# Row-split output matmuls and transposes, and d_ff blocks taken one by one, in a dynamic-convolution and SwiGLU kernel

## The chip, the cores and the metric

The kernel runs on one core of one Trainium2 chip. The time is the device time of one execution in microseconds (us); before the change it was 1409.2 us (median of three runs, 1408.73 to 1409.4).

## What is computed

The reference, cut to what matters:

```python
# x: (4, 4096, 192), weight_gen: (4, 4096, 8 heads, 7 taps)
w = softmax(weight_gen, axis=-1)                 # over the 7 taps
x_pad = six rows of zeros ahead of each sequence
out[b, s, h, g] = sum_k w[b, s, h, k] * x_pad[b, s + k, h*24 + g]
# then, on the 16384 rows of out (d_model 192, d_ff 1536):
xn  = x / sqrt(mean(x*x) + 1e-6) * rms_g
g   = xn @ w_gate ; val = xn @ w_val
return (g * sigmoid(g) * val) @ w_out
```

## The kernel before

**Tiles and blocks.** The 16384 tokens are cut into 32 tiles T of 512 tokens (J = 4 groups of 128). d_ff is cut into FB = 12 blocks f of 128 columns. For each tile and block TensorE does two things:

- `hidden(T, t, f)`, called H(f) below, makes gate and val of the block, transposed: 128 d_ff columns by 512 tokens. The contraction over 192 channels is held in SLOTS = 3 slots of 64 rows, and each operand is split into a high and a low part (float32r), with the three products high-high, low-high, high-low. So H(f) is 9 pairs of matmuls. In each pair the gate matmul uses rows 0 to 63 of the array and the val matmul rows 64 to 127; they write different PSUM banks.
- `project(T, f)`, called P(f), adds the block to the output: for each group j of 128 tokens a matmul of the high part of h with 384 columns (high and low part of w_out side by side) and one of its low part with 192 columns, both over all 128 rows, into the group's own bank of `out_ps`. That is 8 matmuls.

**The chain between them.** ScalarE makes `silu` from gate (L414); VectorE multiplies it with val to h (L538); ScalarE copies the high part `h_hi` (L419); VectorE subtracts to `h_lo` (L556). P(f) waits for `h_lo`. gate and val have two banks each, so H(f+2) waits until h of block f is made.

**Turning x.** Once a tile, `turn_x` transposes the normalised tokens of the next tile on TensorE into a free bank (4 and 2 transposes of 128x128 against the identity). ScalarE copies the high part out (`x_high`, L382 and L385), VectorE the low part (`x_low`, L474 and L478), and three DMAs copy halves between the partitions. The H two blocks later needs that bank again.

**Other work.** VectorE also makes the convolution of the tile after the next in 17 steps (`mix`, two lines L192 and L194 with 0.95 us a step for most), dealt out over the blocks by `steps_other`. ScalarE squares and scales tokens. GpSimd makes 1/rms. In the first tiles VectorE takes the maxima of the remaining taps (L515) and GpSimd subtracts them (L314).

**Order.** Each engine's order is written out by hand, with semaphores; nothing reorders it. On TensorE blocks come in twos: H(f), H(f+1), P(f-2), P(f-1). `turn_x` stands between the two P of f = 4 (`turn_after` is 5). The first H of a tile is followed by H(1), then P(10) and P(11) of the tile before.

Of the kernel before, what the change touches and what calls it, by code (L numbers as in the profile page):

```python
# [5 lines left out]
ALU = mybir.AluOpType  # L6
# [10 lines left out]
def dynconv_swiglu(nc, x, weight_gen, w_gate, w_val, w_out, rms_g, out):  # L17
# [17 lines left out]
    DB = D - DA  # L35
    SLOTS = D // DB
    CHUNKS = ((0, 1, 2), (1, 0, 2))
    FIRST = 3
# [12 lines left out]
    with ExitStack() as ctx:  # L51
# [44 lines left out]
        h = sb("h", [P, 2, N])  # L96
        h_hi = sb("h_hi", [P, 3, N], F32R)
        h_lo = sb("h_lo", [P, 3, N], F32R)
# [42 lines left out]
        h_lo_done = sem("h_lo_done")  # L141
        out_mm_done = sem("out_mm_done")
        out_part_done = sem("out_part_done")
# [9 lines left out]
        def turn_after(T):  # L153


            return 9 if isinstance(T, int) and T == 0 else 5

# [5 lines left out]
        pieces = [slice(a * J * H, b * J * H) for a, b in zip(cuts, cuts[1:])]  # L163

        def rest_to(t, part, odd):

            return xT[0:DB, t, 2, part, :].rearrange("p (j o c) -> p j o c", o=2, c=P)[:, :, odd, :]

        def rest_of(banks, odd):

            return val_ps[odd * DB:odd * DB + DB, banks, 0:N // 2].rearrange("p (j c) -> p j c", c=P)

# [163 lines left out]
        def _(act):  # L336
# [22 lines left out]
            def square(T, t, js):  # L359
                if isinstance(T, int) and T < 2:  # L360
                    act.wait_ge(first_mix, FIRST_DONE)
                    act.wait_ge(pool_mix, CONV * (T + 1))
                else:
                    act.wait_ge(mix_steps, MIX * (T - 1))
                if not (isinstance(T, int) and T == 0):

                    act.wait_ge(mean_done, T)
                    act.wait_ge(xT_done, 2 * T)
# [28 lines left out]
            def out_low(T):  # L397


                act.wait_ge(out_mm_done, FB * (T + 1))  # L400
                nc.scalar.activation(out_part, out_ps[:, :, D:2 * D], ACT.Copy).then_inc(out_part_done, 1)  # L401

            def tile(T, t, first=False, last=False, exps=()):
                xf = turn_after(T)
                squares_at, scales_at = (xf - 4, xf - 3) if first else (0, 2), (xf - 2, xf - 1) if first else (3, 4)
                for f in range(FB):
                    b = pair(t, step_of(f, xf))
                    if f == 2 and not first:
# [5 lines left out]
                    nc.scalar.activation(silu[:, f % 2, :], gate_ps[:, b, :], ACT.Silu).then_inc(silu_done, 1)  # L414
                    act.wait_ge(h_done, FB * T + f + 1)
                    if not (first and f < 3):
# [11 lines left out]
                    if f == xf:  # L428
                        x_high(T + 1, 1 - t, pair(t, xf + 1))
# [16 lines left out]
        def _(dve):  # L446
# [25 lines left out]
            def x_low(T, t, banks):  # L472
                dve.wait_ge(x_hi_done, 3 * T + 1)
                nc.vector.tensor_tensor(xT[:, t, 0, 1, :], gate_ps[:, banks, :], xT[:, t, 0, 0, :].bitcast(F32),  # L474
                                        ALU.subtract).then_inc(x_lo_done, 1)
                for odd in range(2):
                    dve.wait_ge(x_hi_done, 3 * T + 2 + odd)
                    nc.vector.tensor_tensor(rest_to(t, 1, odd), rest_of(banks, odd), rest_to(t, 0, odd).bitcast(F32),  # L478
# [50 lines left out]
            def tile(T, t, i, first=False, mixes=True, last=False):  # L529
                xf = turn_after(T)  # L530
                steps = steps_first if first else steps_other
                for f in range(FB):
                    b = pair(t, step_of(f, xf))
                    if f == 2 and not first:
                        out_add(T - 1, 1 - t, None if isinstance(T, int) and T < 3 else 16 * (i - (1 - t)))
# [7 lines left out]
                    if mixes:  # L543
                        for n in range(sum(steps[:f]), sum(steps[:f + 1])):
# [10 lines left out]
                    dve.wait_ge(h_hi_done, FB * T + f + 1)  # L555
                    nc.vector.tensor_tensor(h_lo[:, f % 3, :], h[:, f % 2, :], h_hi[:, f % 3, :].bitcast(F32),  # L556
                                            ALU.subtract).then_inc(h_lo_done, 1)
                    if f == xf and not last:
                        x_low(T + 1, 1 - t, pair(t, xf + 1))

            tile(0, 0, 0, first=True)
# [11 lines left out]
        def _(pe):  # L573
            def turn_x(T, t, banks):


                pe.wait_ge(xn_done, 2 * J * (T + 1))
                for j in range(J):
                    mm = nc.tensor.transpose(gate_ps[:, banks, j * P:(j + 1) * P], xn_a[:, j, :], ident[:])  # L579
                mm.then_inc(xT_done, 1)  # L580
                for j in range(0, J, 2):
                    mm = nc.tensor.transpose(val_ps[:, banks, j // 2 * P:(j // 2 + 1) * P], xn_b[:, j:j + 2, :].rearrange("p j d -> p (j d)"), ident[:])  # L582
                mm.then_inc(xT_done, 1)
# [44 lines left out]
            def project(T, f):  # L628

                pe.wait_ge(h_lo_done, FB * T + f + 1)  # L630
                for j in range(J):
                    cols = slice(j * P, (j + 1) * P)
                    nc.tensor.matmul(out_ps[:, j, 0:2 * D], h_hi[:, f % 3, cols], wo[:, f, :, :].rearrange("p a d -> p (a d)"),  # L633
                                     start=(f == 0), stop=False, skip_group_check=True)
                    mm = nc.tensor.matmul(out_ps[:, j, 0:D], h_lo[:, f % 3, cols], wo[:, f, 0, :],  # L635
                                          start=False, stop=(f == FB - 1), skip_group_check=True)
                mm.then_inc(out_mm_done, 1)

            def tile(T, t, first=False, last=False):
                xf = turn_after(T)  # L640
                for f in range(0, FB, 2):
                    hidden_waits(T, f, first)
                    hidden(T, t, f)
                    if not (last and f + 1 == xf + 2):
                        hidden_waits(T, f + 1, first)
                    hidden(T, t, f + 1)
                    if f == 0:
                        if not first:
                            project(T - 1, FB - 2)
                            project(T - 1, FB - 1)  # L650
                        continue
                    if f == 2:
# [18 lines left out]
            for _ in range(WARM_TURNS):  # L671
                nc.tensor.transpose(gate_ps[:, 0, 0:P], ident[:], ident[:])
            turn_x(0, 0, 1)
# [30 lines left out]
```

## Time and profile before

| what | value |
|---|---|
| median of 3 runs | 1409.2 us |
| the profiled execution | 1406.67 us, its span 1404.9 us |
| TensorE busy | 1357.4 us, 97% of the span |
| VectorE busy | 996.9 us, 71% |
| ScalarE busy | 659.3 us, 47% |
| mean granted TensorE clock | 0.99 |

The span goes from the first to the last instruction. A matmul's row has a start and a duration; matmuls are pipelined, so the next one starts well before the one before has ended. What a matmul costs a busy TensorE is therefore the distance from its start to the next start. Two matmuls on different halves of the rows start together and count as one step.

### The profile page before, as it was taken

How to read it: one execution, taken by the hardware profiler on the slowest of the kernel's cores; microseconds unless marked ns; L12 is line 12 of the kernel's file. 1: busy time of each engine (PE TensorE's matmuls, PEld its weight loads, DVE VectorE, ACT ScalarE, POOL GpSimd, SP SyncE). 2: the span in 40 equal slices, each digit the busy share in tenths (PEclk: the TensorE clock that was granted, in tenths of full speed). 3: DMA queues.
4: the chain of work that ended last, by engine and by line, in shares of the span. 5: the costliest groups of instructions: out<-in, count | busy, mean ns of one | idle time of the engine just before them, and what ended most of it. 6: DMA issues, size and time to landing. Idle time of an engine off the chain costs nothing.

```text
span 1404.9 us, 27539 instructions
## 1 busy us (share of the span) xinstructions
PE 1357.4 (97%) x10260; PEld 1121.2 (80%) x10260; DVE 996.9 (71%) x1438; ACT 659.3 (47%) x1427; POOL 106.6 (8%) x104
## 2 busy tenths in 40 slices
PE   4898899999999999999999999999999999999998
PEld 3676678888888888888888888888888888888887
DVE  6786777777777777777777777777777777777543
ACT  4354464444444444444444444444444444544443
POOL 7710200000000000000000000000000000000000
PEclk9899999999999999999999999999999999999999
DMA  9121112111211211211211221211121221120010
GB/s 300 24 63 44 42 40 63 51 40 56 62 43 58 62 50 34 62 56 45 62 50 34 62 62 39 62 50 37 59 62 39 62 62 44 40 62 23 22 35 12
DMA packets 20009, 76.19 MB, mean 54 GB/s; under 512 B 3215, under 2 KB 5007, under 8 KB 19854
## 3 DMA queue, kind: packets, MB, share of 16 engines
q1 hardware_dynamic: 19982, 75.83, 18.1%
q8 instruction: 16, 0.26, 0.1%
q14 instruction: 11, 0.09, 0.0%
HBM read 38.07 MB, written 12.58 MB: 36 GB/s over the span
## 4 chain that ended last, share of the span: by engine, by line
PE 92%; DVE 4%; issue 2%; ACT 1%; DMA 1%; POOL 0%; SPq 0%; POOLq 0%; DVEq 0%; ACTq 0%
PE gate_ps L609 56%; PE out_ps L633 23%; PE out_ps L635 9%; PE val_ps L609 2%; PE gate_ps L579 1%; DVE h L538 1%; DVE prod L192 1%; DVE y L194 1%; PE val_ps L582 0%; DVE h_lo L556 0%; DVE tap_max L515 0%; ACT silu L414 0%; ACT xn L377 0%; DMA xT<-xT 0%; DMA taps<-in_weight_gen 0%
## 5 line engine op out<-in xcount | busy, mean ns | idle before, releaser
L609 PE MATMUL gate_ps<-xT,w_hi 64*128 64x512 f32 x2304 | 774.9, 402 | 11.6 <-DMA xT<-xT 5.4
L609 PE MATMUL val_ps<-xT,w_hi 64*128 64x512 f32 x2304 | 775.3, 403 | 0.0
L609 PEld LDWEIGHTS gate_ps<-xT,w_hi 64*128 64x128 f32 x2304 | 427.5, 186 | 137.0 <-issue 33.0
L538 DVE TENSOR_TENSOR h<-val_ps,silu 128x512 f32<-128x512 f32 x384 | 265.1, 690 | 343.3 <-ACT silu L414 343.2
L633 PE MATMUL out_ps<-wo,h_hi 128*128 128x384 f32 x1536 | 474.3, 372 | 0.0
L609 PE MATMUL val_ps<-xT,w_lo 64*128 64x512 f32 x1152 | 453.8, 394 | 0.0
L609 PE MATMUL gate_ps<-xT,w_lo 64*128 64x512 f32 x1152 | 453.4, 394 | 0.0
L609 PEld LDWEIGHTS val_ps<-xT,w_hi 64*128 64x128 f32 x2304 | 427.5, 186 | 0.8
L419 ACT ACTIVATE h_hi<-h 128x512 fp32r<-128x512 f32 x384 | 242.9, 632 | 369.3 <-DVE h L538 369.3
L414 ACT ACTIVATE silu<-gate_ps 128x512 f32<-128x512 f32 x384 | 227.5, 593 | 349.1 <-PE gate_ps L609 339.1
L635 PE MATMUL out_ps<-wo,h_lo 128*128 128x192 f32 x1536 | 385.1, 251 | 0.0
L633 PEld LDWEIGHTS out_ps<-wo,h_hi 128*128 128x128 f32 x1536 | 289.6, 189 | 69.6 <-issue 69.6
L556 DVE TENSOR_TENSOR h_lo<-h,h_hi 128x512 fp32r<-128x512 f32 x384 | 268.8, 700 | 37.2 <-ACT h_hi L419 37.2
L635 PEld LDWEIGHTS out_ps<-wo,h_lo 128*128 128x128 f32 x1536 | 294.3, 192 | 0.0
L609 PEld LDWEIGHTS gate_ps<-xT,w_lo 64*128 64x128 f32 x1152 | 214.4, 186 | 39.0
L609 PEld LDWEIGHTS val_ps<-xT,w_lo 64*128 64x128 f32 x1152 | 214.4, 186 | 0.4
L194 DVE TENSOR_TENSOR y<-y,prod 128x768 f32<-128x768 f32 (+1 forms) x186 | 186.8, 1004 | 2.3
L192 DVE TENSOR_TENSOR prod<-x_buf,tap_w 128x768 f32<-128x768 f32 x180 | 171.1, 951 | 1.1
L283 POOL TENSOR_TENSOR mean_sq<-sq_mean,eps_rms 128x4 f32<-128x4 f32 x32 | 17.6, 550 | 1205.8 <-ACT xn L370 1205.8
L377 ACT ACTIVATE xn<-y,inv_rms 128x128 f32<-128x128 f32 (+1 forms) x256 | 74.0, 360 | 4.4 <-POOL inv_rms L285 4.4
L370 ACT ACTIVATE xn<-y 128x192 f32<-128x192 f32 x128 | 44.4, 348 | 1.7 <-DVE y L194 1.7
L522 DVE TENSOR_TENSOR last<-out_ps,last 128x768 f32<-128x768 f32 x32 | 30.6, 958 | 6.6 <-ACT last L401 3.4
(47 smaller groups left out, 431.9 us busy)
## 6 DMA issues: line engine op xcount, KB each, us to landing
x_buf<-in_x SPq DMA_DIRECT2D x30, 960.0 KB, 4.6
xT<-xT SPq DMA_DIRECT2D x96, 256.0 KB, 3.8
result<-last SPq DMA_DIRECT2D x32, 384.0 KB, 2.3
taps<-in_weight_gen SPq DMA_DIRECT2D x1, 3248.0 KB, 19.5
raw<-in_moe_w_gate SPq DMA_DIRECT2D x3, 384.0 KB, 6.5
raw<-in_moe_w_val SPq DMA_DIRECT2D x3, 384.0 KB, 7.6
last<-in_moe_w_out SPq DMA_DIRECT2D x1, 1152.0 KB, 12.6
x_first<-in_x SPq DMA_DIRECT2D x2, 384.0 KB, 4.9
```

The source lines that it names most:

```text
L192: return engine.tensor_tensor(heads(product if n else acc), heads(flat(src[:, k + j0:k + j1, :])), w[:, q0:q1, k].unsqueeze(2).to_broadcas ...
L194: return engine.tensor_tensor(acc, acc, product, ALU.add)
L370: nc.scalar.activation(xn[:, j * D:(j + 1) * D], y[:, t, j, :], ACT.Square, scale=D ** -0.5, accum_out=sq_mean[:, j:j + 1]).then_inc(squar ...
L377: nc.scalar.activation(part[:, j, :], y[:, t, j, d], ACT.Copy, scale=inv_rms[:, j:j + 1]).then_inc(xn_done, 1)
L414: nc.scalar.activation(silu[:, f % 2, :], gate_ps[:, b, :], ACT.Silu).then_inc(silu_done, 1)
L419: nc.scalar.activation(h_hi[:, f % 3, :], h[:, f % 2, :], ACT.Copy).then_inc(h_hi_done, 1)
L522: nc.vector.tensor_tensor(out_sb[:, t, :, :], out_ps[:, :, 0:D], out_part, ALU.add).then_inc(out_added, 1)
L538: nc.vector.tensor_tensor(h[:, f % 2, :], val_ps[:, b, :], silu[:, f % 2, :], ALU.mult).then_inc(h_done, 1)
L556: nc.vector.tensor_tensor(h_lo[:, f % 3, :], h[:, f % 2, :], h_hi[:, f % 3, :].bitcast(F32), ALU.subtract).then_inc(h_lo_done, 1)
L609: mm = nc.tensor.matmul(ps[:, banks, :], w[rows, s, cols], xT[rows, t, s, part, :], start=(s == 0 and n == 0), stop=ends)
L633: nc.tensor.matmul(out_ps[:, j, 0:2 * D], h_hi[:, f % 3, cols], wo[:, f, :, :].rearrange("p a d -> p (a d)"), start=(f == 0), stop=False, ...
L635: mm = nc.tensor.matmul(out_ps[:, j, 0:D], h_lo[:, f % 3, cols], wo[:, f, 0, :], start=False, stop=(f == FB - 1), skip_group_check=True)
```

## The change

The output matmuls are split in two by rows: rows 0 to 63 of the block go to one group j of tokens and, beside them, rows 64 to 127 to group j + 2, in four turns k = 0 to 3; in turn k + 2 the halves change places. Both halves add into the same bank of `out_ps`, two turns apart, and a new semaphore `bank_left` keeps them apart: turn n waits until all matmuls of turn n - 2 have ended. The transposes are split in the same way (12 instead of 6, with 64 columns each), and write the banks of gate and val, which are now one tensor `up_ps`. Blocks are taken one by one: H(f), P(f-2). `turn_x` moves one block later (`turn_after` is 6), after H(6) and P(4) and ahead of P(5); H(7) then follows without a P between. `h_hi` and `h_lo` have four buffers instead of three. ScalarE's `x_high` stands ahead of the block's `h_hi`, and VectorE's `x_low` ahead of its `h_lo`, and `x_low` now begins after all three copies of `x_high`. Squares, scales, `out_low` and `out_add` come one block earlier.

```diff
+    HB = 4
-        gate_ps = psum("gate_ps", [P, 2, N])
-        val_ps = psum("val_ps", [P, 2, N])
+        up_ps = psum("up_ps", [P, 2, 2, N])
+        gate_ps, val_ps = up_ps[:, :, 0, :], up_ps[:, :, 1, :]
...
-            return 9 if isinstance(T, int) and T == 0 else 5
+            return 9 if isinstance(T, int) and T == 0 else 6
...
             def x_high(T, t, banks):
-                act.wait_ge(xT_done, 2 * T + 1)
-                nc.scalar.activation(xT[:, t, 0, 0, :], gate_ps[:, banks, :], ACT.Copy).then_inc(x_hi_done, 1)
-                act.wait_ge(xT_done, 2 * T + 2)
+                act.wait_ge(xT_done, T + 1)
+                nc.scalar.activation(main_to(t, 0), main_of(banks), ACT.Copy).then_inc(x_hi_done, 1)
...
-                squares_at, scales_at = (xf - 4, xf - 3) if first else (0, 2), (xf - 2, xf - 1) if first else (3, 4)
+                squares_at, scales_at = (xf - 4, xf - 3) if first else (0, 1), (xf - 2, xf - 1) if first else (2, 3)
...
-                        act.wait_ge(out_mm_done, FB * T + f - 2)
-                    nc.scalar.activation(h_hi[:, f % 3, :], h[:, f % 2, :], ACT.Copy).then_inc(h_hi_done, 1)
+                        act.wait_ge(bank_left, 2 * J * (FB * T + f - HB + 1))
+                    nc.scalar.activation(h_hi[:, f % HB, :], h[:, f % 2, :], ACT.Copy).then_inc(h_hi_done, 1)
...
             def x_low(T, t, banks):
-                dve.wait_ge(x_hi_done, 3 * T + 1)
+                dve.wait_ge(x_hi_done, 3 * T + 3)
...
             def turn_x(T, t, banks):
-                pe.wait_ge(xn_done, 2 * J * (T + 1))
                 for j in range(J):
-                    mm = nc.tensor.transpose(gate_ps[:, banks, j * P:(j + 1) * P], xn_a[:, j, :], ident[:])
-                mm.then_inc(xT_done, 1)
...
+                    for m in range(2):
+                        rows = slice(m * DB, (m + 1) * DB)
+                        mm = nc.tensor.transpose(up_ps[:, banks, m, j * DB:(j + 1) * DB], xn_a[rows, j, :], ident[rows, rows])
...
             def project(T, f):
                 pe.wait_ge(h_lo_done, FB * T + f + 1)
-                for j in range(J):
-                    cols = slice(j * P, (j + 1) * P)
-                    nc.tensor.matmul(out_ps[:, j, 0:2 * D], h_hi[:, f % 3, cols], wo[:, f, :, :].rearrange("p a d -> p (a d)"),
-                                     start=(f == 0), stop=False, skip_group_check=True)
-                    mm = nc.tensor.matmul(out_ps[:, j, 0:D], h_lo[:, f % 3, cols], wo[:, f, 0, :],
-                                          start=False, stop=(f == FB - 1), skip_group_check=True)
-                mm.then_inc(out_mm_done, 1)
+                for k in range(J):
+                    turn = J * FB * T + J * f + k
+                    if not (isinstance(turn, int) and turn < 2):
+                        pe.wait_ge(bank_left, 2 * (turn - 1))
+                    for m in range(2):
+                        j = (k + 2 * m) % J
+                        rows, cols = slice(m * DB, (m + 1) * DB), slice(j * P, (j + 1) * P)
+                        nc.tensor.matmul(out_ps[:, j, 0:2 * D], h_hi[rows, f % HB, cols],
+                                         wo[rows, f, :, :].rearrange("p a d -> p (a d)"),
+                                         start=(f == 0 and k < 2), stop=False, skip_group_check=True)
+                    for m in range(2):
+                        j = (k + 2 * m) % J
+                        rows, cols = slice(m * DB, (m + 1) * DB), slice(j * P, (j + 1) * P)
+                        nc.tensor.matmul(out_ps[:, j, 0:D], h_lo[rows, f % HB, cols], wo[rows, f, 0, :], start=False,
+                                         stop=(f == FB - 1 and k >= 2), skip_group_check=True).then_inc(bank_left, 1)
...
-                for f in range(0, FB, 2):
-                    hidden_waits(T, f, first)
-                    hidden(T, t, f)
...
-                    project(T, f - 2)
-                    if f + 1 == xf and not last:
...
-                        turn_x(T + 1, 1 - t, pair(t, xf + 1))
-                    project(T, f - 1)
+                for f in range(FB):
...
+                    if 2 <= f <= xf or f > xf + 1:
+                        project(T, f - 2)
+                    if f == xf:
+                        if not last:
+                            turn_x(T + 1, 1 - t, pair(t, xf + 1))
+                        project(T, xf - 1)
```

TensorE's queue before, where H of a tile's block 5 ends and P(2) begins (L609 is H, L633 and L635 are P, L577 to L582 belong to `turn_x`; the names in brackets are the semaphores waited for):

```order
L609 MATMUL gate_ps<-xT,w_hi 128x512
L609 MATMUL val_ps<-xT,w_hi 128x512
L633 MATMUL out_ps<-wo,h_hi 128x384 [waits h_lo_done]
L635 MATMUL out_ps<-wo,h_lo 128x192
L633 MATMUL out_ps<-wo,h_hi 128x384
```

The queue of the changed kernel, where an H ends and a P begins, up to its turn k = 2 (L619 is H, L649 and L655 are P; ISA is a register instruction):

```order
L619 MATMUL up_ps<-xT,w_hi 128x512 x2
L645 ISA [waits h_lo_done]
L649 MATMUL out_ps<-wo,h_hi 128x384 [waits bank_left]
L649 MATMUL out_ps<-wo,h_hi 128x384
L655 MATMUL out_ps<-wo,h_lo 128x192 x2
L645 ISA
L649 MATMUL out_ps<-wo,h_hi 128x384 [waits bank_left]
L649 MATMUL out_ps<-wo,h_hi 128x384
L655 MATMUL out_ps<-wo,h_lo 128x192 x2
L645 ISA
L649 MATMUL out_ps<-wo,h_hi 128x384 [waits bank_left]
```

Four matmuls now stand where two stood, and each turn begins with a wait of TensorE for its own earlier matmuls.

ScalarE's queue before, around the copies of the turned x of a tile (L382, L385):

```order
L414 ACTIVATE silu<-gate_ps 128x512 [waits h_done,gate_done]
L419 ACTIVATE h_hi<-h 128x512 [waits out_mm_done,h_done]
L382 ACTIVATE xT<-gate_ps 128x512 [waits xT_done]
L385 ACTIVATE xT<-val_ps 64x2x128 [waits xT_done]
L385 ACTIVATE xT<-val_ps 64x2x128
```

The same place of the changed kernel (L391, L393):

```order
L422 ACTIVATE silu<-up_ps 128x512 [waits h_done,gate_done]
L391 ACTIVATE xT<-up_ps 128x512 [waits xT_done]
L393 ACTIVATE xT<-up_ps 64x2x128 x2
L429 ACTIVATE h_hi<-h 128x512 [waits bank_left,h_done]
L422 ACTIVATE silu<-up_ps 128x512 [waits h_done,gate_done]
```

The copies of x have moved ahead of the copy of h, and wait for all transposes at once.

## Rows read from the trace of the kernel before

**Rows 1.** The profile page, busy time and share of the engines.
```profile
PE 1357.4 (97%) x10260; PEld 1121.2 (80%) x10260; DVE 996.9 (71%) x1438; ACT 659.3 (47%) x1427; POOL 106.6 (8%) x104
```

**Rows 2.** The chain that ended last, by engine (page).
```profile
PE 92%; DVE 4%; issue 2%; ACT 1%; DMA 1%; POOL 0%; SPq 0%; POOLq 0%; DVEq 0%; ACTq 0%
```

**Rows 3.** Busy time in one tile's stretch: us, then busy (count) per engine, clock, DMA.
```profile
686.33:728.08 41.75, 41.75 (x321) 34.53 (x319) 30.40 (x46) 19.77 (x44) 1.53 (x2) 1.00 0.17 52
```

**Rows 4.** Timeline of TensorE, end of a P, start of an H: start, us.
```profile
702.28 0.25 PE L635 MATMUL out_ps<-wo,h_lo 128*128 128x192 f32 x1
702.46 0.49 PE L609 MATMUL gate_ps<-xT,w_hi 64*128 64x512 f32 x1
...
702.80 0.39 PE L609 MATMUL gate_ps<-xT,w_lo 64*128 64x512 f32 x1
...
703.03 0.40 PE L609 MATMUL gate_ps<-xT,w_hi 64*128 64x512 f32 x1
```

**Rows 5.** Timeline of TensorE, end of an H, start of a P.
```profile
706.53 0.39 PE L609 MATMUL gate_ps<-xT,w_hi 64*128 64x512 f32 x1
...
706.86 0.45 PE L633 MATMUL out_ps<-wo,h_hi 128*128 128x384 f32 x1
707.14 0.25 PE L635 MATMUL out_ps<-wo,h_lo 128*128 128x192 f32 x1
707.23 0.36 PE L633 MATMUL out_ps<-wo,h_hi 128*128 128x384 f32 x1
707.42 0.25 PE L635 MATMUL out_ps<-wo,h_lo 128*128 128x192 f32 x1
```

**Rows 6.** Timeline of TensorE around the transposes of x.
```profile
708.00 0.25 PE L635 MATMUL out_ps<-wo,h_lo 128*128 128x192 f32 x1
708.08 0.60 PE L579 MATMUL gate_ps<-ident,xn 128*128 128x128 f32 x4
708.52 0.38 PE L582 MATMUL val_ps<-ident,xn 128*128 128x128 f32 x2
708.66 0.42 PE L633 MATMUL out_ps<-wo,h_hi 128*128 128x384 f32 x1
```

**Rows 7.** Timeline of weight loads at the start of an H.
```profile
702.46 0.18 PEld L609 LDWEIGHTS gate_ps<-xT,w_hi 64*128 64x128 f32 x1 [0.16 <-issue]
702.47 0.18 PEld L609 LDWEIGHTS val_ps<-xT,w_hi 64*128 64x128 f32 x1
702.57 0.19 PEld L609 LDWEIGHTS gate_ps<-xT,w_lo 64*128 64x128 f32 x1
702.57 0.19 PEld L609 LDWEIGHTS val_ps<-xT,w_lo 64*128 64x128 f32 x1
```

**Rows 8.** Timeline where TensorE is woken by another engine (tile 0).
```profile
78.11 0.86 DVE L478 TENSOR_TENSOR xT<-val_ps,xT 64x256 fp32r<-64x256 f32 x2
...
79.03 0.18 PEld L609 LDWEIGHTS gate_ps<-xT,w_hi 64*128 64x128 f32 x1 [1.26 <-DVE xT L478]
```

**Rows 9.** The same in tile 1, with a wait for two semaphores.
```profile
130.46 0.69 DVE L538 TENSOR_TENSOR h<-val_ps,silu 128x512 f32<-128x512 f32 x1 [3.91 <-ACT silu L414]
...
131.27 0.18 PEld L609 LDWEIGHTS gate_ps<-xT,w_hi 64*128 64x128 f32 x1 [2.12 <-ACT silu L414]
```

**Rows 10.** Timelines of ScalarE, VectorE and TensorE after a turn of x.
```profile
709.69 0.58 ACT L382 ACTIVATE xT<-gate_ps 128x512 fp32r<-128x512 f32 x1
710.16 0.77 ACT L385 ACTIVATE xT<-val_ps 64x256 fp32r<-64x256 f32 x2
...
710.50 0.68 DVE L474 TENSOR_TENSOR xT<-gate_ps,xT 128x512 fp32r<-128x512 f32 x1
711.10 0.86 DVE L478 TENSOR_TENSOR xT<-val_ps,xT 64x256 fp32r<-64x256 f32 x2
...
712.16 0.40 PE L609 MATMUL gate_ps<-xT,w_hi 64*128 64x512 f32 x1
```

**Rows 11.** The chain that ended last in tile 1: start, us, what.
```profile
97.07 2.86 DVE tap_max L515
...
100.86 5.43 issue
```

**Rows 12.** The stretch at half clock in tile 1, columns as in Rows 3.
```profile
107.40:114.30 6.90, 4.85 (x20) 4.40 (x22) 5.15 (x9) 3.93 (x10) 0.00 (x0) 0.51 0.00 0
```

More of the change, by code:

```diff
@@ L96, in dynconv_swiglu @@
         h = sb("h", [P, 2, N])
-        h_hi = sb("h_hi", [P, 3, N], F32R)
-        h_lo = sb("h_lo", [P, 3, N], F32R)
+        h_hi = sb("h_hi", [P, HB, N], F32R)
+        h_lo = sb("h_lo", [P, HB, N], F32R)
         out_part, out_sb = last[:, 0, :, :], last[:, 1:3, :, :]
-        gate_ps = psum("gate_ps", [P, 2, N])
-        val_ps = psum("val_ps", [P, 2, N])
+        up_ps = psum("up_ps", [P, 2, 2, N])
+        gate_ps, val_ps = up_ps[:, :, 0, :], up_ps[:, :, 1, :]
         out_ps = psum("out_ps", [P, J, N])
@@ L367, in square @@
                     act.wait_ge(mean_done, T)
-                    act.wait_ge(xT_done, 2 * T)
+                    act.wait_ge(xT_done, T)
                 for j in js:
@@ L404, in tile @@
                 xf = turn_after(T)
-                squares_at, scales_at = (xf - 4, xf - 3) if first else (0, 2), (xf - 2, xf - 1) if first else (3, 4)
+                squares_at, scales_at = (xf - 4, xf - 3) if first else (0, 1), (xf - 2, xf - 1) if first else (2, 3)
                 for f in range(FB):
                     b = pair(t, step_of(f, xf))
-                    if f == 2 and not first:
+                    if f == 1 and not first:
                         out_low(T - 1)
@@ L414, in tile @@
                     nc.scalar.activation(silu[:, f % 2, :], gate_ps[:, b, :], ACT.Silu).then_inc(silu_done, 1)
+                    if f == xf and not last:
+                        x_high(T + 1, 1 - t, pair(t, xf + 1))
                     act.wait_ge(h_done, FB * T + f + 1)
-                    if not (first and f < 3):
-                        act.wait_ge(out_mm_done, FB * T + f - 2)
-                    nc.scalar.activation(h_hi[:, f % 3, :], h[:, f % 2, :], ACT.Copy).then_inc(h_hi_done, 1)
+                    if not (first and f < HB):
+                        act.wait_ge(bank_left, 2 * J * (FB * T + f - HB + 1))
+                    nc.scalar.activation(h_hi[:, f % HB, :], h[:, f % 2, :], ACT.Copy).then_inc(h_hi_done, 1)
                     if last:
@@ L427, in tile @@
                         scale(T + 1, 1 - t, range(2 * n, 2 * n + 2))
-                    if f == xf:
-                        x_high(T + 1, 1 - t, pair(t, xf + 1))
                     for at, n in exps:
@@ L533, in tile @@
                     b = pair(t, step_of(f, xf))
-                    if f == 2 and not first:
+                    if f == 1 and not first:
                         out_add(T - 1, 1 - t, None if isinstance(T, int) and T < 3 else 16 * (i - (1 - t)))
@@ L554, in tile @@
                             mix(T + 2, t, n)
-                    dve.wait_ge(h_hi_done, FB * T + f + 1)
-                    nc.vector.tensor_tensor(h_lo[:, f % 3, :], h[:, f % 2, :], h_hi[:, f % 3, :].bitcast(F32),
-                                            ALU.subtract).then_inc(h_lo_done, 1)
                     if f == xf and not last:
                         x_low(T + 1, 1 - t, pair(t, xf + 1))
+                    dve.wait_ge(h_hi_done, FB * T + f + 1)
+                    nc.vector.tensor_tensor(h_lo[:, f % HB, :], h[:, f % 2, :], h_hi[:, f % HB, :].bitcast(F32),
+                                            ALU.subtract).then_inc(h_lo_done, 1)
             tile(0, 0, 0, first=True)
@@ L574, in turn_x @@
             def turn_x(T, t, banks):
-                pe.wait_ge(xn_done, 2 * J * (T + 1))
                 for j in range(J):
-                    mm = nc.tensor.transpose(gate_ps[:, banks, j * P:(j + 1) * P], xn_a[:, j, :], ident[:])
-                mm.then_inc(xT_done, 1)
-                for j in range(0, J, 2):
-                    mm = nc.tensor.transpose(val_ps[:, banks, j // 2 * P:(j // 2 + 1) * P], xn_b[:, j:j + 2, :].rearrange("p j d -> p (j d)"), ident[:])
+                    for m in range(2):
+                        rows = slice(m * DB, (m + 1) * DB)
+                        mm = nc.tensor.transpose(up_ps[:, banks, m, j * DB:(j + 1) * DB], xn_a[rows, j, :], ident[rows, rows])
+                for q in range(J // 2):
+                    for m in range(2):
+                        rows = slice(m * DB, (m + 1) * DB)
+                        mm = nc.tensor.transpose(up_ps[:, banks, m, N // 2 + q * DB:N // 2 + (q + 1) * DB],
+                                                 xn_b[rows, 2 * q:2 * q + 2, :].rearrange("p j d -> p (j d)"), ident[rows, rows])
                 mm.then_inc(xT_done, 1)
@@ L639, in tile @@
             def tile(T, t, first=False, last=False):
                 xf = turn_after(T)
-                for f in range(0, FB, 2):
-                    hidden_waits(T, f, first)
+                for f in range(FB):
+                    if not (last and f == xf + 2):
+                        hidden_waits(T, f, first)
                     hidden(T, t, f)
[L644 to L651, printed above, removed]
+                    if f == 0 and not first:
+                        project(T - 1, FB - 2)
+                        project(T - 1, FB - 1)
@@ L657, in tile @@
                             pe.wait_ge(w_lo_done, SLOTS + 1)
-                    project(T, f - 2)
-                    if f + 1 == xf and not last:
+                    if f == xf and not last:
                         pe.wait_ge(silu_done, FB * T + xf)
                         pe.wait_ge(h_done, FB * T + xf)
-                        turn_x(T + 1, 1 - t, pair(t, xf + 1))
-                    project(T, f - 1)
+                        pe.wait_ge(xn_done, 2 * J * (T + 2))
+                    if 2 <= f <= xf or f > xf + 1:
[4 more added lines that the diff above has]
+                        project(T, xf - 1)
             pe.wait_ge(consts_done, 1)
@@ L671, in _ @@
             for _ in range(WARM_TURNS):
-                nc.tensor.transpose(gate_ps[:, 0, 0:P], ident[:], ident[:])
+                nc.tensor.transpose(up_ps[:, 0, 0, 0:P], ident[:], ident[:])
+            pe.wait_ge(xn_done, 2 * J)
             turn_x(0, 0, 1)
```

16 lines of the change are left out of this document (10 added, 6 removed).

## The prediction

> **What bounds the kernel now.** I read the page's busy times first: TensorE is busy for 97% of the span, VectorE for 71%, ScalarE for 47% [rows 1]. The chain that ended last says the same: 92% of the span goes through TensorE [rows 2]. One tile in the steady part takes 41.75 us, at full clock, and TensorE has no idle time in it, while VectorE works 30.40 us and ScalarE 19.77 us [rows 3]. So the time is what TensorE's instructions cost from start to start, and the other engines matter only where they make it wait. That happens in the first tiles (below).
>
> Now the steps, from start to start. Inside an H a pair takes 0.233 us: one starts at 702.80, the next at 703.03, and from 702.80 to the last pair at 706.53 there are 16 steps [rows 4, 5]. Inside a P the step after an h_hi matmul is 0.19 and after an h_lo matmul 0.09; from 707.14 to 708.00 three groups of tokens pass, 0.286 each [rows 5, 6]. Transposes and the step into them show nothing extra: 0.08 after the h_lo matmul at 708.00, and about 0.65 us for all six, of which 0.58 lie between 708.08 and 708.66 [rows 6]. So a tile should need 12 x 9 x 0.233 = 25.2, 12 x 4 x 0.286 = 13.7, and 0.65: 39.5 us. It takes 41.75. The missing 2.2 us are at the borders between H and P, of which there are six there and six back in a tile. Going to H: 0.18 instead of 0.09, then 0.34 instead of 0.233 [rows 4]. Going to P: 0.33 instead of 0.233, then 0.28 instead of 0.19 [rows 5]. Together 0.38 us for a round trip, and 2.2 / 6 = 0.37 from the tile. What is special there is that the number of rows changes, 64 to 128 or back. P to transposes and back, 128 rows throughout, shows none of it, and neither does H to H.
>
> **The change, part by part.**
>
> *Borders.* With P and the transposes on 64 rows, no border between different row counts is left. I take the whole 2.2 us off each tile: 32 x 2.2 = 70.4 us. That there are now 12 round trips a tile instead of 6 then costs nothing. The Trainium skill says, in TensorEngine Tiling (Array Packing), Tiling Modes, that changing the tiling mode drains TensorE. The trace agrees in the place of the gaps; the skill gives no time for it.
>
> *The split matmuls.* A P had 8 matmuls and 8 loads, now 16 and 16, in 8 steps of two. Columns per step are as before. What must hold is that the loads and matmuls of two row halves run side by side also when the steps are as short as 0.09. H shows matmuls side by side, but its steps are long. For the loads the best rows are the start of an H: gate and val load at 702.46 and 702.47, and the next two both at 702.57, so two loads per half, four in all, start within 0.11 us [rows 7]. Had they gone through one port one by one, the second pair would start at 0.2 and 0.3 us. I take 0.286 for a turn, as before. The bound on the good side is the same; on the bad side it is a rival below.
>
> *The wait for the bank.* Turn n waits for all of turn n - 2. The second h_lo matmul of a turn starts 0.01 after the first and lasts 0.25 [rows 5]; TensorE's load starts 0.06 after the end of the VectorE instruction that it waits for (78.11 + 0.86 = 78.97, load at 79.03) [rows 8]. So turn k + 2 can load 0.32 after turn k's h_lo step starts. Without the wait its load would stand at the start of turn k + 1's h_lo step, 0.286 later. It is 0.034 late at least. In a P that follows an H, turns 0 and 1 wait for turns long past; turn 2 pays, and turn 3 hardly, since turn 1 is judged against a stream that turn 2 has already set back. So one payment a block. I take 0.06 us, as the rows are rounded, two semaphore counts must arrive and a register instruction stands ahead of each wait: 384 x 0.06 = 23 us. The bounds: nothing (0 us), if the queue holds enough, and 0.12 us with the dearer wake of [rows 9], where 131.15 to 131.27 is 0.12 and not 0.06, plus 0.03 for refilling: 46 us. Queued behind a waiting turn are only TensorE's own matmuls. By the Trainium skill, TensorE: Matmul & The Clock Gate, Part 3 on the per-tile semaphore tail, each further increment adds 26.3 ns; an estimate with it is 0.034 + 0.026 = 0.06 us a block. No row here shows that figure.
>
> *Blocks one by one.* H(f+2) needs h of block f. Between the end of H(f) and the start of H(f+2) now lie P(f-2), H(f+1) and P(f-1), 1.2 + 2.1 + 1.2 = 4.5 us, while silu and h take 0.6 and 0.69 and a short wait for the matmul's end: covered by some 2 us even when VectorE first finishes a 0.95 step and an h_lo. P(f) comes after H(f+2), later still. VectorE's 30.4 us [rows 3] lie inside a tile of 40.3 us. I cost this at nothing. Without its cover it would cost what the VectorE is late, up to a step of 0.95 a block.
>
> *The turned x.* H(8) needs the low part of x. From the first transpose: 0.82 to the end of the last (708.52 + 0.38 - 708.08) [rows 6]; then x_high 1.24 (709.69 to 710.93) and, now only after it, x_low 0.60 + 0.86 = 1.46 [rows 10]; with three hand-overs of 0.05, 3.65 us. Before, ScalarE began 1.61 after the first transpose, held by h_hi, and the low part was done at 711.96, 0.20 ahead of the H at 712.16 [rows 10]. H(8) now starts 0.65 + 4 x 0.286 + 0.06 + 9 x 0.233 = 3.95 us after the first transpose. The slack stays, 0.3 us. I cost it at nothing; if the copies, whose pieces are now 64 columns wide, took 30% longer, 0.8 us, H(8) would be 0.5 late in 31 tiles: 16 us. The halves' DMAs have the rest of the tile. In tile 0 x_low starts about 0.7 later and the first H with it.
>
> *The first tiles.* In tiles 1 and 2 a reduction of 2.86 us and then 5.43 us in which VectorE stands still hold up h, and through h the normalised x [rows 11]; the transposes wait 6 us and the clock is 0.51 for 6.9 us afterwards [rows 12]. These waits are set by VectorE and GpSimd, and P(3) will meet them instead of the transposes. One block less has been issued ahead of it, but P(3) needs less than the transposes did. Between -2 and +8 us, I take 2 us gained in all.
>
> *Sum.* Against the profiled execution: 1406.7 - 70.4 + 23 - 2 = 1357.3 us. The median is 2.5 above that execution, so 1360 us, a tile of 12 x (2.10 + 1.14 + 0.06) + 0.65 = 40.3 us.
>
> **The rivals.**
>
> *The wait is free.* The queue is deep enough and the wake quick: the 23 us are not paid, perhaps more is won in the first tiles: 1337 us. For it: only 0.034 us is missing. Against: the load cannot start before its wait ends.
>
> *The wait is dear,* or every border to H refills TensorE's queue, or H(8) is late: 0.12 to 0.17 a block, 46 to 65 us instead of 23: 1383 to 1402 us. For it: 16 instructions, register steps and waits now share 1.2 us.
>
> *The short steps don't run side by side.* Place: each turn of P. If the two halves' loads take turns, the h_lo step lasts two loads, 2 x 0.11 = 0.22 instead of 0.09, and the h_hi step 0.22 instead of 0.19: 0.16 more a turn, 384 x 4 x 0.16 = 246 us: 1360 + 246, about 1606 us. It decides from (70.4 - 23 + 2) / 1536 = 0.03 us a turn. Against it stand the loads of [rows 7]; for it, that no row shows steps under 0.23 with two halves.
>
> *The borders are not of the row count* but of any change from H to P, for instance queue refills. Then 12 round trips instead of 6 cost 70 us more: 1409 + 70 + 23 = 1502 us. Against it: the borders at the transposes cost nothing.
>
> *VectorE's latency shows.* Stalls of 0.5 to 2 us a tile: 1376 to 1420 us. A tile leaves VectorE 10 us free [rows 3], so I hold it small.
>
> **How the numbers follow.** Forecast 0.54 (its own range 1346 to 1380); wait free 0.15; wait dear 0.13; not side by side 0.07; borders remain 0.04; VectorE's latency 0.07, half of that still faster. Faster by over 0.2% (which is about what a measurement of this kernel can tell) is 0.54 + 0.15 + 0.13 + 0.04 = 0.86; slower 0.12; same 0.02. The range that holds eight in ten takes in the first three cases, from 1334 (all of the wait free, 2 us more in the first tiles) to 1395.
>
> **What the profile after would show.** Right: starts across a border 0.23 and 0.09 apart; a turn of 0.286 from turn 0 to 1 and some 0.06 more into turn 2; a tile of 40.3 us with no TensorE idle time; H(8) right after H(7). Wrong: turns over 0.32 from the first on (halves not side by side); 0.33 at H to P as now (borders not of the row count); VectorE or ScalarE as releasers of H(8), or of H in every tile; a second gap at the P to H border (queue refill).

## The result, and the profile after

The changed kernel takes 1415.1 us (median of five runs, 1413.1 to 1416.0) against 1408.7 us before: a ratio of 1.0045, 95% interval 1.003 to 1.006. It is slower by half a per cent, where 1360 us had been forecast. Its profiled execution has a span of 1411.3 us. All ratios here and below are taken from executions in the faster of two states; one execution of experiment 5 fell in the slower one, with 1401.9 us at a mean granted clock of 0.845, and is not counted.

The page, lines that answer to [rows 1], and the queue that fetches instructions:

```profile
PE 1319.6 (94%) x13524; PEld 1146.7 (81%) x13524; DVE 1002.0 (71%) x1438; ACT 660.3 (47%) x1427; POOL 97.2 (7%) x104
...
q8 instruction: 138, 2.26, 0.7%
```

TensorE has more instructions than before (13524 matmuls instead of 10260), less busy time, and is now idle for 6% of the span instead of 3%. The last line (packets, MB, share) had 16 packets and 0.26 MB before.

First the part that was forecast. TensorE's timeline from the last pair of an H through a P into the next H, which answers to [rows 4, 5] (start, us):

```profile
701.65 0.40 PE L619 MATMUL up_ps<-xT,w_hi 64*128 64x512 f32 x2
701.89 0.34 PE L649 MATMUL out_ps<-wo,h_hi 64*128 64x384 f32 x2
702.06 0.25 PE L655 MATMUL out_ps<-wo,h_lo 64*128 64x192 f32 x2
702.15 0.36 PE L649 MATMUL out_ps<-wo,h_hi 64*128 64x384 f32 x2
702.35 0.25 PE L655 MATMUL out_ps<-wo,h_lo 64*128 64x192 f32 x2
702.43 0.41 PE L649 MATMUL out_ps<-wo,h_hi 64*128 64x384 f32 x2
702.68 0.25 PE L655 MATMUL out_ps<-wo,h_lo 64*128 64x192 f32 x2
702.77 0.36 PE L649 MATMUL out_ps<-wo,h_hi 64*128 64x384 f32 x2
702.97 0.25 PE L655 MATMUL out_ps<-wo,h_lo 64*128 64x192 f32 x2
703.05 0.42 PE L619 MATMUL up_ps<-xT,w_hi 64*128 64x512 f32 x2
703.31 0.39 PE L619 MATMUL up_ps<-xT,w_lo 64*128 64x512 f32 x2
...
706.33 0.42 PE L619 MATMUL up_ps<-xT,w_hi 64*128 64x512 f32 x2
```

H to P takes 0.24 us, where it took 0.33; P to H 0.08 and then 0.26, where it took 0.18 and 0.34. Turns 0 and 1 take 0.26 and 0.28. Turn 2 begins on time at 702.43, but its first step lasts 0.25 instead of 0.20: its load, at 702.40, starts 0.05 after the h_lo matmuls of 702.35, where turn 1's load, at 702.07, starts 0.01 after those of 702.06. A block takes 3.28 us, from the H at 703.05 to the one at 706.33; 3.30 had been forecast. A tile without a pause takes 39.89 us at full clock (the same pair of H starts at 313.71 and, a tile later, at 353.60), with TensorE busy throughout. The first row below covers all but 0.09 us of it and answers to [rows 3]; the one after it answers to [rows 12]:

```profile
314.00:353.80 39.80, 39.80 (x422) 34.56 (x420) 30.64 (x45) 19.77 (x44) 1.21 (x2) 1.00 0.12 31
394.80:398.90 4.10, 3.75 (x20) 3.37 (x22) 0.00 (x0) 0.00 (x0) 0.00 (x0) 0.60 0.49 204
```

Now the part that was not. Every second tile ends like this:

```profile
391.33 0.36 PE L649 MATMUL out_ps<-wo,h_hi 64*128 64x384 f32 x2
391.53 0.25 PE L655 MATMUL out_ps<-wo,h_lo 64*128 64x192 f32 x2
395.15 0.50 PE L619 MATMUL up_ps<-xT,w_hi 64*128 64x512 f32 x2 [3.37 <-issue]
395.46 0.56 PE L619 MATMUL up_ps<-xT,w_lo 64*128 64x512 f32 x2
```

TensorE stands still for 3.37 us, and no other engine or DMA of the program is named as releaser, that is, as what ended the wait ("issue" stands there instead). Behind most of these pauses the clock is at its lower level for 3.4 us or twice that: 0.60 is the mean of the stretch above. The profile's list of waits counts the pauses (us in total, times, longest):

```profile
PE up_ps L619 <- issue: 44.3, 13, 3.7
```

Thirteen pauses, 44.3 us, 3.7 at most. Thirteen is the number of times that TensorE's loop over pairs of tiles jumps back. The instructions at the source line of the loop show the jump itself. PEldq is the sequencer that feeds TensorE, COMPARE_BRANCH the jump (count: shortest, median, longest in ns). In the kernel before:

```profile
L676 PEldq COMPARE_BRANCH  x14: 76/208/242, 227.1 to 1312.7; - x14
```

and in the changed kernel:

```profile
L696 PEldq COMPARE_BRANCH  x14: 83/3422/3777, 222.8 to 1323.4; - x14
```

Thirteen jumps of 3.3 to 3.8 us, the last one (not taken) 0.08. Before the change they took 0.21, and TensorE did not stand still: its queue still held matmuls. Counted in the traces, the loop's body on TensorE had 1333 instructions before (636 loads, 636 matmuls, 61 others) and has 1839 now (840, 840, and 159, of which 96 are the register instructions ahead of the bank waits).

**Theory A:** the body no longer stays in TensorE's instruction store, the memory into which its instructions are fetched, and each jump back waits until its first instructions have been fetched again; with the clock that is what ate the gain. **Theory B:** the pause belongs to the new order or to a wait for another engine at the start of a pair of tiles, and the long branch only covers it.

### The profile page after: what moved, and what is told of

Read it like the earlier page. It is cut to its first block, busy times and chain, and to the rows that moved or that the text cites. A ratio compares the mean times of both kernels' runs of the same rounds, so it can differ in the third digit from the quotient of the medians.

```text
span 1411.3 us, 35391 instructions
## 1 busy us (share of the span) xinstructions
PE 1319.6 (94%) x13524; PEld 1146.7 (81%) x13524; DVE 1002.0 (71%) x1438; ACT 660.3 (47%) x1427; POOL 97.2 (7%) x104
## 4 chain that ended last, share of the span: by engine, by line
PE 88%; issue 4%; DVE 4%; ACT 3%; DMA 1%; POOL 0%; SPq 0%; ACTq 0%; POOLq 0%
PE up_ps L619 57%; PE out_ps L649 21%; PE out_ps L655 9%; DVE h L545 1%; ACT silu L422 1%; DMA xT<-xT 1%; DVE prod L201 1%; PE up_ps L587 1%; DVE y L203 1%; DVE tap_max L522 0%; ACT taps L403 0%; ACT xn L386 0%; DVE h_lo L565 0%; DMA taps<-in_weight_gen 0%; PE up_ps L591 0%
## 5 line engine op out<-in xcount | busy, mean ns | idle before, releaser
L619 PE MATMUL up_ps<-xT,w_hi 64*128 64x512 f32 x4608 | 800.4, 402 | 53.9 <-issue 44.3
L619 PEld LDWEIGHTS up_ps<-xT,w_hi 64*128 64x128 f32 x4608 | 445.4, 188 | 146.3 <-issue 48.5
L649 PE MATMUL out_ps<-wo,h_hi 64*128 64x384 f32 x3072 | 488.2, 370 | 12.7 <-DVE h_lo L565 12.7
L545 DVE TENSOR_TENSOR h<-up_ps,silu 128x512 f32<-128x512 f32 x384 | 265.3, 691 | 300.0 <-ACT silu L422 292.1
L619 PE MATMUL up_ps<-xT,w_lo 64*128 64x512 f32 x2304 | 464.3, 397 | 0.0
L422 ACT ACTIVATE silu<-up_ps 128x512 f32<-128x512 f32 x384 | 227.9, 594 | 377.5 <-PE up_ps L619 375.4
L655 PE MATMUL out_ps<-wo,h_lo 64*128 64x192 f32 x3072 | 391.1, 250 | 0.0
L649 PEld LDWEIGHTS out_ps<-wo,h_hi 64*128 64x128 f32 x3072 | 295.8, 187 | 42.5 <-issue 8.7
L655 PEld LDWEIGHTS out_ps<-wo,h_lo 64*128 64x128 f32 x3072 | 298.6, 189 | 13.8
L619 PEld LDWEIGHTS up_ps<-xT,w_lo 64*128 64x128 f32 x2304 | 223.9, 189 | 36.5
L391 ACT ACTIVATE xT<-up_ps 128x512 fp32r<-128x512 f32 x32 | 19.2, 599 | 30.7 <-PE up_ps L591 30.7
```

What stands on the lines that cost most here:

```text
L545: nc.vector.tensor_tensor(h[:, f % 2, :], val_ps[:, b, :], silu[:, f % 2, :], ALU.mult).then_inc(h_done, 1)
L619: mm = nc.tensor.matmul(ps[:, banks, :], w[rows, s, cols], xT[rows, t, s, part, :], start=(s == 0 and n == 0), stop=ends)
L649: nc.tensor.matmul(out_ps[:, j, 0:2 * D], h_hi[rows, f % HB, cols], wo[rows, f, :, :].rearrange("p a d -> p (a d)"), start=(f == 0 and k < ...
L655: nc.tensor.matmul(out_ps[:, j, 0:D], h_lo[rows, f % HB, cols], wo[rows, f, 0, :], start=False, stop=(f == FB - 1 and k >= 2), skip_group_ ...
```

## The experiments

**1. The loop written out.** Edit on the changed kernel:

```diff
-            with pe.Fori(1, TILES // 2 - 1) as i:
+            for i in range(1, TILES // 2 - 1):
                 tile(2 * i, 0)
```

> The changed kernel with TensorE's loop over pairs of tiles written out in full (the other engines keep their loops). Theory A (code fetch): the 13 taken branches back, 3.3 to 3.8 us each, and the stretch at half clock behind each, some 1.6 us, are the cost of fetching the first instructions of a loop body that no longer fits. Without a branch both go: 13 x 5.1 = 67 us less than the changed kernel, 1348 us, no gap over 1 us between the H of tiles 4 and 28. Theory B (a wait for another engine or a DMA at the start of an odd-even pair of tiles): the gap stays, the time stays at 1415 us.

Measured: 1352.9 us, ratio to the kernel before 0.9599 (0.9583 to 0.9616). The pauses are gone; all tiles from 3 on take 40.13 us. Its fetch queue moves 108 packets, 1.77 MB, nearly as much as in the changed kernel, and nothing waits: straight code is fetched ahead, so the traffic is not the cost. Theory B falls; the size of the body, theory A's reason, is tested in experiments 3, 8 and 9.

**2. The loop kept, with a hint:** one instruction at the loop's top that names the jump back and its target.

```diff
-            with pe.Fori(1, TILES // 2 - 1) as i:
+            with nc.Fori(1, TILES // 2 - 1, engines=[mybir.EngineType.PE], hint_back_edge=True) as i:
```

> The changed kernel, its loop kept, with one hint instruction at the top of TensorE's loop that names the branch back and its target. Theory A: the first instructions of the body are fetched ahead, the branch takes 0.2 to 0.5 us as in the kernel before, and the time is 1348 to 1356 us. Theory B: no change, 1415 us.

Measured: 1359.6 us, ratio 0.9645 (0.9628 to 0.9661). The branch and the fetch queue of this run:

```profile
L696 PEldq COMPARE_BRANCH  x14: 80/216/253, 219.9 to 1268.1; - x14
```

```profile
q8 instruction: 21, 0.34, 0.1%
```

The body has 1840 instructions, one more than the changed kernel's, and the branch takes 0.22 us. More than that: 21 packets instead of 138. With the hint the body is not fetched again at all: in the trace no packet starts between 202 and 1269 us, from the loop's first pass to the end of its last. So it does fit as a whole, and lack of room is not the full story.

The packets say more. The unrolled kernel's 27821 instructions on TensorE come in 108 packets, some 258 each. The changed kernel's 138 - 21 = 117 packets more are nine for each of the 13 jumps, and nine start between each jump and the next in its trace. In experiment 8 below it is nine as well, though a body of 1765 instructions can touch eight at most. So at least one packet a pass must lie outside the loop, most simply behind its end. That this fetching ahead replaces the loop's beginning, and that the hint stops it, is the likely reading; no run shows it. Against the unrolled kernel 6.7 us are left; at the jumps the last step of the odd tiles is 0.4 us longer, 13 times, some 5 us, which is most of it.

**3. The kernel before with a longer body.** Waits for semaphores that were reached long before, ahead of each matmul in the loop; the lines for H, and the same ahead of both matmuls of P:

```diff
                             rows = slice(m * DB, (m + 1) * DB)
+                            if not isinstance(T, int):
+                                for waited in (w_hi_done, w_lo_done):
+                                    pe.wait_ge(waited, 1)
                             mm = nc.tensor.matmul(ps[:, banks, :], w[rows, s, cols], xT[rows, t, s, part, :],
```

> The kernel before, its matmuls and order unchanged, with already satisfied semaphore waits added ahead of the matmuls in the loop: about 620 more instructions on TensorE in two tiles, some 1950 instead of 1334 (the changed kernel has about 1840). Theory A (size of the body alone): the branch back takes 3.3 to 3.8 us 13 times and costs with the clock 55 to 70 us: 1465 to 1480 us. Theory B (something in the split matmuls or the new order): no stall, 1409 us; should the waits themselves slow TensorE's issue, every H gets longer, and the trace shows which.

Measured: 1567.1 us, ratio 1.1114 (1.1095 to 1.1133), with a body of 1957 instructions:

```profile
L685 PEldq COMPARE_BRANCH  x14: 76/3325/3896, 232.5 to 1475.1; - x14
L612 PE MATMUL gate_ps<-xT,w_hi 64*128 64x512 f32 x2304 | 825.4, 421 | 86.2 <-issue 74.0
q8 instruction: 148, 2.42, 0.6%
```

The branch does what theory A says, in a kernel whose matmuls and order are those of before. The time is 90 us above the expectation. TensorE pauses 26 times and not 13, for 74.0 us in all: 3 to 4 us behind the start of TensorE's work after each jump comes a second one of 1.7 to 2.8 us. The time at half clock costs 46 us more than in the kernel before, and most of the last 38 of the 158 us lies in H blocks that became longer (two H take 4.76 to 4.98 us instead of 4.39 or 4.40). For the second pauses and for the longer H the added waits and the fetching can't be told apart in this run.

**4. The new order alone, over 128 rows.** The changed kernel with P and the transposes as before:

```diff
-                for k in range(J):
-                    turn = J * FB * T + J * f + k
...
+                for j in range(J):
+                    cols = slice(j * P, (j + 1) * P)
+                    nc.tensor.matmul(out_ps[:, j, 0:2 * D], h_hi[:, f % HB, cols], wo[:, f, :, :].rearrange("p a d -> p (a d)"),
+                                     start=(f == 0), stop=False, skip_group_check=True)
+                    nc.tensor.matmul(out_ps[:, j, 0:D], h_lo[:, f % HB, cols], wo[:, f, 0, :],
+                                     start=False, stop=(f == FB - 1), skip_group_check=True).then_inc(bank_left, 2)
```

> The changed kernel's order (blocks one by one, transposes after H(6), four h buffers) with the output matmuls and transposes over 128 rows as before. If the 0.37 us of a round trip belong to a change between 64 and 128 rows, 10 round trips a tile instead of 6 cost 4 x 0.37 = 1.5 us a tile, 48 us in all: 1457 us. If they belong to any change between H and P, the same, and then the changed kernel should show them too. The loop body is as short as before, so by theory A the branch back takes 0.2 us; by theory B, if the order is to blame, 3.4 us remain.

Measured: 1450.6 us (1457 expected), ratio 1.0285 (1.0268 to 1.0302). Its timeline from an H to the next (start, us):

```profile
704.71 0.39 PE L612 MATMUL up_ps<-xT,w_hi 64*128 64x512 f32 x2
705.04 0.44 PE L636 MATMUL out_ps<-wo,h_hi 128*128 128x384 f32 x1
705.32 0.25 PE L638 MATMUL out_ps<-wo,h_lo 128*128 128x192 f32 x1
...
706.18 0.25 PE L638 MATMUL out_ps<-wo,h_lo 128*128 128x192 f32 x1
706.36 0.50 PE L612 MATMUL up_ps<-xT,w_hi 64*128 64x512 f32 x2
706.70 0.40 PE L612 MATMUL up_ps<-xT,w_lo 64*128 64x512 f32 x2
```

The borders cost what they cost before: 0.33 and 0.28 into P, 0.18 and 0.34 into H. A tile takes 43.28 us, 1.53 more than before, which is four round trips at 0.38. The changed kernel has as many transitions between H and P, none of them between row counts, and shows none of this cost. So the borders cost by the change of rows, and over 128 rows the new order makes the kernel 41 us slower. Its branch, with a body of 1335 instructions, takes 0.21 us; the order is not to blame for the pauses.

**5. The bank wait taken off the path.** The unrolled changed kernel, each P cut in half; the first half stands behind an H, the second inside the next one:

```diff
+            owed = []
+            def pay():
+                if owed:
+                    project_half(*owed.pop(), 1)
+            def project(T, f):
+                pay()
+                project_half(T, f, 0)
+                owed.append((T, f))
...
-                for k in range(J):
+                for k in (2 * half, 2 * half + 1):
...
                 for s in range(SLOTS):
+                    if s == 2:
+                        pay()
```

> The unrolled changed kernel with each P cut in half: turns 0 and 1 stand behind an H, turns 2 and 3 inside the next H, after its sixth pair. No work is added. Each turn then waits for turns that ended long before. If the bank wait is what makes turn 2 start late (0.055 us in the changed kernel's trace, 12 times a tile), a tile falls from 40.13 to 39.5 us and the time by 32 x 0.6 = 19 us, to 1334 us. The rival, that the delay belongs to the pace at which TensorE's queue is fed, or that a border between H and P costs something even without a change of rows: there are now twice as many borders, and the time stays at 1353 us or rises.

Measured: 1343.9 us (1334 expected), ratio 0.9524 (0.951 to 0.9537). Its timeline where six turns stand in a row behind a tile's first H, and then at a half of P inside an H:

```profile
703.28 0.41 PE L662 MATMUL out_ps<-wo,h_hi 64*128 64x384 f32 x2
703.52 0.26 PE L668 MATMUL out_ps<-wo,h_lo 64*128 64x192 f32 x2
...
703.82 0.25 PE L668 MATMUL out_ps<-wo,h_lo 64*128 64x192 f32 x2
703.96 0.44 PE L662 MATMUL out_ps<-wo,h_hi 64*128 64x384 f32 x2
704.21 0.28 PE L668 MATMUL out_ps<-wo,h_lo 64*128 64x192 f32 x2
...
705.77 0.41 PE L621 MATMUL up_ps<-xT,w_hi 64*128 64x512 f32 x2
706.01 0.36 PE L662 MATMUL out_ps<-wo,h_hi 64*128 64x384 f32 x2
706.18 0.27 PE L668 MATMUL out_ps<-wo,h_lo 64*128 64x192 f32 x2
706.27 0.38 PE L662 MATMUL out_ps<-wo,h_hi 64*128 64x384 f32 x2
706.47 0.28 PE L668 MATMUL out_ps<-wo,h_lo 64*128 64x192 f32 x2
706.55 0.44 PE L621 MATMUL up_ps<-xT,w_hi 64*128 64x512 f32 x2
706.81 0.41 PE L621 MATMUL up_ps<-xT,w_lo 64*128 64x512 f32 x2
```

In a half inside an H no step of 0.25 after an h_hi pair is left, and twice as many borders cost next to nothing. A tile takes 39.62 us instead of 40.13. The 0.51 us are four fifths of what was expected, and the timeline shows why: the edit does not separate all turns. Steps some 0.05 too long, 14 in a tile of the unrolled changed kernel, are still 5 here: three where six turns stand in a row (0.24 and 0.25 after h_hi, 0.14 after h_lo) and two where four follow the transposes. With 29 tiles the gain is 15 us. The first three tiles gave 5 of them back (151.9 us against 146.6).

**6. The kernel before, unrolled**, by the edit of experiment 1.

> The kernel before with TensorE's loop written out in full. Its branch back takes 0.21 us in the trace and is covered by the queue. If unrolling helps the changed kernel only by its stalled branches, nothing changes here: 1408 to 1410 us. If straight code is faster by itself, this falls too, by up to 10 us.

Measured: 1408.3 us, ratio 0.999 (0.9981 to 1.0). Unrolling by itself brings at most 0.2%.

**7. Split output matmuls, blocks still in twos.** The kernel before, unrolled, with the changed kernel's `project` (three h buffers) and its bank waits; transposes over 128 rows.

> The kernel before, unrolled, with only the output matmuls split by rows and the bank waits: blocks stay in twos, the transposes stay over 128 rows, three h buffers. The borders of H and P lose their 0.37 us, those of P and the transposes gain it once a tile, and 8 turns in a row pay the bank wait about four times in two blocks instead of two: 39.5 + 0.4 + 1.0 = 40.9 us a tile against 40.1, 32 x 0.8 = 26 us over the unrolled changed kernel: 1378 us. The rival, that taking blocks one by one is what brings the gain: then this stays near 1405 us.

Measured: 1390.9 us (1378 expected), ratio 0.9873 (0.9856 to 0.989). A tile takes 41.07 us (40.9 expected), and the first three take 155.0 us. So what this run leaves out (blocks one by one, split transposes, the fourth h buffer) adds 38 us to the gain of the split. The profiled executions are 34 us apart: 27 us in the later tiles (0.94 us in each of 29, of which the transposes' own border is about 0.4 and the longer runs of turns, with four steps some 0.05 too long in two blocks, the rest) and 8 us in the first three, less 2 elsewhere. The three parts were not tested one by one.

**8 and 9. How long a body may be.** The kernel of experiment 3 with the waits ahead of H's matmuls only, and then ahead of every second of them.

> As the kernel with the lengthened body, but with satisfied waits ahead of H's matmuls only: about 1766 instructions in TensorE's body, between the 1334 of before and the 1840 of the changed kernel. The duration of the branch back brackets the size: 0.2 us, and the limit lies above 1766; or 3.3 us and more, and it lies between 1334 and 1766. The time itself also contains what the added waits cost.

Measured: 1503.1 us (one run), with a body of 1765 instructions:

```profile
L679 PEldq COMPARE_BRANCH  x14: 83/3641/3866, 232.0 to 1409.1; - x14
L612 PE MATMUL gate_ps<-xT,w_hi 64*128 64x512 f32 x2304 | 801.7, 414 | 61.9 <-issue 48.2
q8 instruction: 134, 2.20, 0.6%
```

> Half as many satisfied waits: about 1550 instructions in TensorE's body. With 1766 the branch back took 3.3 to 3.9 us, with 1334 0.2 us. If the room is what decides, this one brackets it: 0.2 us, and the limit lies between 1550 and 1766; or above 3 us, and it lies between 1334 and 1550. By the Trainium skill (Runtime: NRT & Kernel Launch, Instruction fetch mechanics), TensorE holds 2048 instructions in blocks of 256, which alone would let all three bodies fit.

Measured: 1407.6 us (one run), with 1549 instructions:

```profile
L679 PEldq COMPARE_BRANCH  x14: 83/215/243, 227.9 to 1313.5; - x14
q8 instruction: 17, 0.28, 0.1%
```

The limit lies between 1549 and 1765. In the last kernel nothing is fetched between the first jump and the last, and 216 added waits cost nothing at all. That the waits of experiment 8, twice as many, cost little by themselves is likely but not shown: its blocks away from the jump are mostly as long as before. TensorE stands still for 48 us around the 13 jumps, in two pauses each, and is at half clock for 78 us more than in the kernel before, of which half is lost: 48 + 39 of the 94 us.

**10. The best version:** experiment 5 with whole P in tiles 0 to 2.

```diff
                 owed.append((T, f))
+                if T < 3:
+                    pay()
```

> As the kernel with the bank wait hidden, but in tiles 0 to 2, where other engines hold TensorE up, each P stays whole. In the run with halves everywhere these three tiles took 151.9 us, in the unrolled changed kernel 146.6. If the halves make the first tiles' waits longer, 5 us come back: 1339 us. If the first tiles vary by themselves, 1344 us.

Measured: 1340.2 us, ratio 0.9507 (0.9494 to 0.952): 4.9% faster than the kernel before and 5.3% faster than the changed kernel. The first three tiles take 148.7 us, so 3 of the 5 us came back. Since two executions of experiment 5 took 1340.7 and 1340.9 us, the step from 5 to 10 in the whole time is not sure.

## Why the prediction was wrong

- **The borders of H and P:** right. The rows had shown that only a change of rows costs; experiment 4 puts 1.53 us on four more round trips, and the changed kernel has none of them. The 70 us were there to be had. That TensorE drains at a change of tiling mode, as the Trainium skill says in TensorEngine Tiling (Array Packing), Tiling Modes, agrees with this.
- **Split matmuls side by side in short steps:** right, 0.28 to 0.29 us a turn without a late load. The rival that had put the time at 1606 us fell with it.
- **The bank wait:** right in its place (turn 2 pays, turn 3 doesn't), with 0.05 us at the step where 0.06 was taken. One payment a block was forecast, 12 x 0.06 = 0.72 us a tile; the unrolled kernel has 14 steps some 0.05 too long, and experiment 5, which takes away nine of them, gains 0.51 us.
- **Blocks one by one, the turned x:** right. No H of a steady tile waits for another engine. The hand-overs of the turned x add up to 3.67 us and not to 3.65, which changes nothing. The first three tiles take 146.6 us in the unrolled kernel's profile against 154.8 before, about 2 us better than forecast; but they take 149.9 in the changed kernel's own profile, so the 2 us may be chance.
- **The sum:** for a kernel without jumps, 1360 us was forecast and 1352.9 us measured. Most of the difference is the steady tile, 40.13 us instead of 40.3.
- **What failed** is a term that isn't in the sum. The step "The split matmuls" counts 16 matmuls and 16 loads where 8 and 8 stood and prices only their time in the array; "the wait" adds a register instruction to each turn. The prediction never asked where the 500 new instructions of two tiles are kept. They made the loop's body 1839 instructions long, and 13 jumps back cost 1415.1 - 1352.9 = 62 us: 44.3 us of pauses, and 19 us of half clock behind ten of them (nine stretches of 3.4 us and one of 6.8, of which half is lost); together 63. That the two agree this closely is in part luck: in the profiled executions the changed kernel's first three tiles also take 3 us more than the unrolled one's, and the loop's other tiles are some 0.2 us shorter than the unrolled kernel's, for which no run gives the reason. The 56 us gained by everything else went into this, and 6 us more. The forecast list of what would show it wrong had "a second gap at the P to H border", but as a slow refill of the queue in each block, at 0.05 us.
- The size was there to read. The kernel before has a TensorE loop of two tiles; 20520 loads and matmuls in 32 tiles are some 1280 in its body, and the changed kernel's code gives 1680 plus a register instruction per turn. The Trainium skill, Runtime: NRT & Kernel Launch, Instruction fetch mechanics, says that TensorE's store holds 2048 instructions in blocks of 256, and that a taken branch whose target is not in the current 2-page window stalls until it is fetched. The stall agrees with the runs. The sizes agree only in part: without a hint 1765 instructions already stall, with one 1840 stay inside, and jumps back over 1333 and 1549 instructions, which is more than two pages, are free.

## What to carry to other kernels

When a change splits instructions in a loop, count the instructions of the body on that engine before and after, not only their time; a jump back that was free became 3.4 us of pause here, with half clock behind most of them. Look at the branch's own duration and at the packets of the instruction queue: both are in the profile and point at the cause at once. And a gap that belongs to switching between 64 and 128 rows can be told from the transitions that don't switch; to be rid of it was worth 4% here, net of what the split cost.

## What the hardware showed that was not expected

- A TensorE loop of 1333 to 1549 instructions jumps back in 0.21 us; one of 1765 to 1957 in 3.3 to 3.9 us. With a hint at the top of the loop 1840 instructions jump back in 0.22 us, and the fetch queue falls from 138 packets to 21.
- Where the jump stalls, more is fetched in each pass than the loop can hold: nine packets of some 258 instructions for a body of 1765.
- Straight code of 27000 loads and matmuls, 1.77 MB fetched, made TensorE wait nowhere in the steady tiles.
- After 10 of the 13 pauses of some 3.4 us, in an engine that had been busy for 80 us, the granted clock fell from 2.4 to 1.2 GHz for 3.4 us or more.
